# Attention on one core: the sixteen-row matmul of the pooled values is given all 128 rows

## The reference, cut to what matters

```python
q_d = q.reshape(B, H, Sd, factor, D).mean(axis=3)      # B 4, H 8, Sd 144, factor 4, D 64
k_d = k.reshape(B, H, Sd, factor, D).mean(axis=3)
v_d = v.reshape(B, H, Sd, factor, D).mean(axis=3)
out_d = sm_attn(q_d, k_d, v_d)                         # softmax(q k^T / 8) v
out_up = np.repeat(out_d, factor, axis=2)
...
mask = np.abs(pos[:, None] - pos[None, :]) < factor    # the local half
...
return (out_up + out_local).astype(np.float32)
```

## Time and profile before

| | |
|---|---|
| time before, 3 runs | 711.68, 711.68 and 710.21 us (median 711.68) |
| profiled execution, its own time | 710.25 us |
| its span in the trace | 708.5 us |
| granted TensorE clock | full speed (1.00) in all stretches |
| PE matmul busy | 691.6 us, 98% of the span |
| PE weight loads busy | 630.8 us, 89% |
| DVE, ACT, POOL busy | 368.3, 261.2, 185.5 us |
| attention rounds with L647 | from 16.0 to 102.3 us |
| L647 | 128 matmuls and 128 weight loads |

### The profile page before, as it was taken

One profiled execution on the slowest core, in us unless ns is written; L12 is line 12 of the kernel. 1 busy time (PEld: TensorE's weight loads), 2 busy tenths in 40 slices (PEclk: granted clock), 3 DMA queues, 4 the chain that ended last, 5 costly groups with the idle time before them and its releaser, 6 DMA issues.

```text
span 708.5 us, 12646 instructions
## 1 busy us (share of the span) xinstructions
PE 691.6 (98%) x5098; PEld 630.8 (89%) x5098; DVE 368.3 (52%) x688; ACT 261.2 (37%) x583; POOL 185.5 (26%) x228
## 2 busy tenths in 40 slices
PE   5999999999999999999999999999989999999998
PEld 4777779999999999999999999999768888888886
DVE  8898867642233223322232322564796667756671
ACT  4887864332112211221121122135564544444441
POOL 5999920000000000000000000584535434354100
PEclk9999999999999999999999999999999999999999
DMA  7788783000000000000000030002100000000001
GB/s 232 227 224 236 212 310 145 1 0 1 1 1 1 0 1 1 1 1 0 1 1 1 1 118 1 1 1 73 47 16 16 30 31 16 15 31 31 30 16 44
DMA packets 25657, 37.51 MB, mean 53 GB/s; under 512 B 2944, under 2 KB 13184, under 8 KB 25472
## 3 DMA queue, kind: packets, MB, share of 16 engines
q1 hardware_dynamic: 25600, 36.72, 16.4%
HBM read 31.99 MB, written 4.72 MB: 52 GB/s over the span
## 4 chain that ended last, share of the span: by engine, by line
PE 91%; DVE 3%; POOL 2%; issue 2%; ACT 1%; DMA 1%; SPq 0%; DVEq 0%; ACTq 0%; POOLq 0%
PE psum L690 28%; PE psum L676 28%; PE psum L783 12%; PE psum L760 11%; PE psum L647 3%; PE psum L769 2%; PE psum L662 1%; PE psum L593 1%; PE psum L627 1%; PE psum L636 1%; PE psum L612 1%; DMA kT<-kT_dram 1%; POOL ylo L554 1%; DVE so L1298 1%; PE psum L606 0%
## 5 line engine op out<-in xcount | busy, mean ns | idle before, releaser
L1195 DVE CAST ghi<-g_sb 128x384 fp32r<-128x384 f32 x96 | 39.6, 412 | 245.3 <-PE psum L690 188.5
L899 ACT ACTIVATE g_sb<-psum 128x384 f32<-128x384 f32 x96 | 47.0, 490 | 292.4 <-PE psum L676 288.2
L676 PE MATMUL psum<-xhi,whi 128*128 128x384 f32 x384 | 129.6, 338 | 1.7 <-ACT g_sb L899 0.8
L676 PE MATMUL psum<-xhi,wlo 128*128 128x384 f32 x384 | 129.0, 336 | 0.0
L676 PE MATMUL psum<-xlo,whi 128*128 128x384 f32 x384 | 129.0, 336 | 0.0
L690 PE MATMUL psum<-ghi,wlo 128*128 128x384 f32 x384 | 129.0, 336 | 0.0
L690 PE MATMUL psum<-ghi,whi 128*128 128x384 f32 x384 | 129.0, 336 | 0.0
L690 PE MATMUL psum<-glo,whi 128*128 128x384 f32 x384 | 129.0, 336 | 0.0
L526 POOL TENSOR_TENSOR t<-raw 128x1024 f32<-128x1024 f32 x1 | 2.6, 2614 | 351.5 <-PE psum L690 351.5
L676 PEld LDWEIGHTS psum<-xhi,whi 128*128 128x128 f32 x384 | 72.2, 188 | 2.8 <-ACT g_sb L899 1.3
L690 PEld LDWEIGHTS psum<-ghi,whi 128*128 128x128 f32 x384 | 72.2, 188 | 0.1
(11 more groups left out here) (123 smaller groups left out, 1072.3 us busy)
## 6 DMA issues: line engine op xcount, KB each, us to landing
wraw<-w_dram SPq DMA_DIRECT2D x12, 512.0 KB, 6.9
qT<-qT_dram SPq DMA_DIRECT2D x16, 288.0 KB, 3.7
kT<-kT_dram SPq DMA_DIRECT2D x16, 288.0 KB, 5.1
out_dram<-ob SPq DMA_DIRECT2D x18, 256.0 KB, 2.0
v<-v_dram SPq DMA_DIRECT2D x16, 256.0 KB
vw<-v_dram SPq DMA_DIRECT2D x32, 128.0 KB, 3.5
wraw<-w_dram SPq DMA_DIRECT2D x16, 256.0 KB, 5.8
raw<-w_dram SPq DMA_DIRECT2D x1, 2048.0 KB, 7.4
```

The lines of the kernel that those rows point to most:

```text
L676: ins = nc.tensor.matmul(bank, a[:, w], b[:, kdx, :], start=(kdx == 0 and n == 0), stop=(kdx == KD - 1 and n == 2))
L899: nc.scalar.activation(g_sb[:, f % HR, :], psum[:, HB1 + f % HB, 0:N1], ACT.Mish).then_inc(g_ok, 1)
L1195: nc.vector.tensor_copy(ghi[:, f % GR, :], g_sb[:, f % HR, :]).then_inc(ghi_ok, 1)
```

## The change

`value_pooled` multiplies group 1 over all 128 partitions of `vd` and `pprobT` in place of its first 16. The rows that are added are zero on both sides. The number of instructions, their order on every engine, the 144 columns that each streams, the tiles in PSUM and all waits stay as they are; the operands of two instructions in each round are wider.

```diff
                 for h in range(2):
                     rows = slice(h * HD, (h + 1) * HD)
-                    for g, n in enumerate((P, PT)):
-                        ins = nc.tensor.matmul(turned[rows, OD0:OD0 + POOLED], vd[0:n, par, g, rows],
-                                               pprobT[0:n, g, :, h, :], start=(g == 0), stop=(g == 1))
+                    for g in range(2):
+                        ins = nc.tensor.matmul(turned[rows, OD0:OD0 + POOLED], vd[:, par, g, rows],
+                                               pprobT[:, g, :, h, :], start=(g == 0), stop=(g == 1))
                 ins.then_inc(p_valued, 1)
```

## The result

Over 20 executions of each kernel the median went from 709.26 to 707.38 us; the ratio of after to before is 0.9967, 95% interval 0.9952 to 0.9981. The fastest executions are 708.54 and 705.54 us, 3.0 apart. The profiled execution took 705.66 us with a span of 703.9, 4.6 less than the profiled one of before, which was not among its fastest (710.25 against 708.54).

What follows compares the result with a forecast made beforehand. PE, 98% busy, was taken to bound the kernel; 4 s in quiet rounds, 0.5 us odd to even and 2 s at the end give 3.4, taken as 711.0 - 3.3 = 707.7 us; range 705.4 to 710.0.

Steps and rivals of the forecast that it cites:

- The break: L647: each change between 128 and 16 rows loses 0.146 us on PE, four times; the change removes three.
- Rival 1: L647's idle time comes with every new product, whatever its rows: saving 0, 711.0 us; every load showing, 710.1; chance 0.10.
- s: The saving in one L647: 0.49 us, with 0.43 and 0.55 as bounds.
- at most that is one step, 0.12 ... I take half: L647, between the heads: head 1's first step overlaps head 0's last, at most 0.12 us, taken as 0.06.
- an L647 of 1.06 to 1.12 us in the chain: Sign expected in the chain of work: L647 takes 1.06 to 1.12 us in place of 1.55.
- Even to odd, quiet: Rounds 2, 6, 10, 14: a ring through L647, DVE having 0.65 us of slack, passes s whole, four times.
- Even to odd with `split_x`: Rounds 4, 8, 12: DVE works without idle time, so an earlier `exp_local` finds it busy; saving 0.
- Odd to even: POOL's run without L647 sets the path: 0, but 0.09 us in rounds 6 and 14; 0.5 together with round 10.
- rival 4: Slower: DVE's short operations fall into POOL's `half_v` in odd rounds too, 0.4 us each; 712.4 us, chance 0.04.
- Round 10: Odd to even, where a 0.43 us break within L593 made it later than `vd`: up to 0.34 us gained.
- The end: Rounds 16 and 17 have their L647 in the chain, and what follows hangs on L662: twice s.
- rival 3: Rings give less: POOL and DVE collide, or `vw` or weights late in round 14; 1 to 2 us, chance 0.15.

Runs made afterwards that it cites:

- mixed: Kernel before, with group 1 of head 0 alone over 128 rows, head 1 keeping 16; 1.02 us from first L647 to first L662.
- short_head: Changed kernel without head 1's second product, its last 16 pooled keys left out; 0.64 us from L647 to L662.
- ten: Kernel before, with 128 rows in group 1 only in rounds 3, 4, 5, 7, 8, 9, 11, 12, 13, 15; first L690 at 107.7 us, before 108.4.
- rows32: Group 1 over 32 rows, in place of 16 in the kernel before or 128 in the changed one; 708.5 us, one execution.
- after_again: The changed kernel measured a second time, nothing altered; ratio to before 0.9951 (0.9933 to 0.9968).
- rows64: Group 1 over 64 rows, in place of 16 in the kernel before or 128 in the changed one; 708.1 us, one execution.
- evict_act: Changed kernel with the second eviction of the local values moved from DVE to ACT; ratio to before 0.9985 (0.9971 to 0.9999).
- light_after: Changed kernel with POOL relieved: group 1's values not pooled, last 16 pooled keys left out; ratio to before 0.9969 (0.9952 to 0.9985).
- rows96: Group 1 over 96 rows, in place of 16 in the kernel before or 128 in the changed one; 708.1 us, one execution.
- light_before: Kernel before with POOL relieved: group 1's values not pooled, last 16 pooled keys left out; ratio to before 0.9973 (0.9955 to 0.9992).

## Why the prediction was right, and where it was not

**The break.** Right: it belongs to the change of row size. Three of four vanished, L636's pace was the proper pattern, and the rule that it cited from the Trainium skill (TensorEngine Tiling (Array Packing), Tiling Modes, Key Properties) agrees with the row counts tried: beside 128 rows 16, 32 and 64 break, 96 doesn't. Rival 1, by which every step would show its load and L647 would take 1.46 us, is out: it took 0.72.

**s.** The term "at most that is one step, 0.12 ... I take half" was mis-sized: s measured 0.9, not 0.49. I reasoned that head 1's first step could at best overlap head 0's last, because its product stands behind in the program. In fact head 1's four steps run beside head 0's four: in the changed kernel eight loads take 0.48 us, and mixed and short_head show the same. What had kept the heads apart before was also the change of row size between them. So the sign that it gave, an L647 of 1.06 to 1.12 us in the chain, was missed by far: it is 0.65.

**Even to odd, quiet.** "DVE has 0.65 of slack: s passes whole" would have held for 0.49 and did not for 0.9: the distance fell by 0.55 in rounds 6, 10 and 14 (5.43 to 4.88), near the slack, and by 0.87 in round 2, where DVE had 0.96. The size of the cap was in the earlier trace rows; what makes it is the wait of `exp_local` for DVE's L1114. ACT's wait for L647 fell from 0.97 to 0.34 us and not "by little": L647 left the ring.

**Even to odd with `split_x`.** 0 forecast, 0.05 measured; ten shows the same with those L647 alone.

**Odd to even.** 0.09 forecast in the quiet pairs; it was 0.02 longer. After the quiet rounds (7 to 8, 11 to 12) the distance grew by 0.28, and from 3 to 4 by 0.12, which was not in the sum. The 0.28 is the collision of rival 4 in a small size: L1128 took 0.46 in place of 0.16, so that `rden`, and with it POOL's run, came 0.3 later than `kd` and L647. The prediction said that POOL and DVE would shift together; they did not, as POOL doesn't start its run on `kd`.

**Round 10.** Up to 0.34 forecast; 0.62 was had, as the break inside L593 didn't occur in this trace. It isn't a gain of the change: ten, whose other distances are those of before, doesn't have it either.

**The end.** "Twice s" was 0.98, with one more s for round 14; measured from round 14's L647 to the first L690 it is 2.6. Round 14 gave 0.55 and round 17 0.9. Round 16 gave only 0.38 between 16 and 17, as DVE's weights became its limit. From 15 to 16 0.79 came unforeseen: DVE's L1159, 1.76 us in the chain before, took 0.68. That is not the change's either: in rows32, whose L647 is that of before, it took 0.68 too and the distance was 5.85, while ten had 1.75 and 6.92, and `after_again`, the changed kernel, 1.75. The timelines show what decides it: where POOL's L503 is under way when L1159 starts (86.74 and 86.98 in before; ten and `after_again` alike), L1159 ends 0.55 us after L503 does; where L1159 starts first (84.72 and 84.79 in after, rows32 alike), it takes 0.68.

**The sum.** 3.4 forecast and 4.6 in the two profiled executions, of which 0.6 is the break and some 1.1 L1159; that leaves 2.9, and rows32, free of both, has a span of 706.8 against 703.9, 2.9 more as well. The fastest executions are 3.0 apart, the ratio says 2.3. It came out near because errors met: s was too small, its cap and the longer odd to even distances were not in the sum. That 707.7 us stands so near the measured 707.38 is luck besides: the forecast started from 711.0, where the median of before is 709.26, and took off 3.3, where the medians are 1.9 apart. What separates 3.0 from 2.3 is, as far as the traces show it, what rival 3 named, `vw` late in round 14, and the clock behind it. Of the 20 executions of after, six had a mean clock of 0.995 and took 707.6 to 711.5 us; of the nine at 1.00 eight took 705.5 to 706.7. The kernel before has executions below 1.00 as well, 21 of the 51 that ran beside the experiments, but only three of these at 0.995.

## What to carry to other kernels

Matmuls of different row size one behind the other (16, 32 or 64 rows beside 128; 96 counts as 128) cost a break each, here 0.15 us, and don't overlap even where they lie in different column halves. Pad the small one with zero rows to the size of its neighbours, or group the products by row size; both gave the same here. Then look at who else has work in the ring: a step that is 0.9 us shorter sixteen times gave 3 us, since only four rounds and the two last passed it on. The idle time in front of the next instruction is the slack only as long as nothing else ends just before: here it was DVE waiting for ACT, and ACT in turn was bound to an earlier step of DVE. And a trace of before may hold delays of its own (1.7 us here), which a difference of two traces then counts as gain.

## What the runs showed of the hardware that was not expected

- Products of the two column halves ran side by side though all of one stood ahead of the other in the program: eight loads in 0.48 us, and 0.64 to 0.65 from L647 to L662 with eight steps as with six. In rows64 seven matmuls of L662 start before L647's last.
- A 64-row product lets the loads of the 64-row products behind it start beside it (L662 at 65.08, together with L647's last product).
- An idle time of PE of 2.7 us in the attention was followed by a granted clock of 0.50, in which six transposes took 1.38 us in place of 0.79; so it was after 2.7 us in short_head, 3.3 in evict_act and 4.3 in light_after. In rows96 PE was idle for 3.1 us at the same place and the clock stayed at 1.00, so the length of one idle time doesn't decide it. Light_after, in which PE idles more, had a mean clock below 1.00 in eight of ten executions; light_before in none of ten, the kernel before beside them in seven of 19.
- An addition of 13 columns on DVE (L1128) takes 0.16 us or, if POOL is within an instruction when it starts, lasts until that ends: 0.25 to 0.92 us in rounds 3 to 14 of the traces of before and after. L1105 and L1121 run beside POOL's instructions at their usual length.
